# VectorE block transposes and a round trip through memory in place of TensorE transposes, in a fused windowed-attention and feed-forward kernel

## The reference

```python
# x: (4, 4096, 192), weight_gen: (4, 4096, 8 heads, 7 taps), moe_w_in: (192, 2048), moe_w_out: (2048, 192), all float32
w = softmax(weight_gen, axis=-1)                     # over the 7 taps, with 1e-9 added to the sum
attn[b, s, h, g] = sum_k w[b, s, h, k] * x_padded[b, s + k, h, g]   # x_padded: 6 zero rows ahead of each sequence
t = attn.reshape(16384, 192)
h = t @ w_in
out = (h * clip(h + 3, 0, 6) / 6) @ w_out
```

## Time and profile before

| what | value |
|---|---|
| three runs | 1182.89, 1185.61, 1186.64 us (median 1185.61) |
| the profiled execution | 1178.76 us, its span 1177.0 us |
| mean granted TensorE clock | 0.998 |
| busy: PE, PEld, DVE, ACT, POOL | 1162.3, 1089.3, 813.2, 662.0, 676.1 us |
| DMA | 42.34 MB, mean 36 GB/s |
| chain that ended last | PE 95% |

### The profile page before, as it was taken

One profiled execution on the slowest core, in us unless ns is written; L12 is line 12 of the kernel. 1 busy time (PEld: TensorE's weight loads), 2 busy tenths in 40 slices (PEclk: granted clock), 3 DMA queues, 4 the chain that ended last, 5 costly groups with the idle time before them and its releaser, 6 DMA issues.

```text
span 1177.0 us, 33989 instructions
## 1 busy us (share of the span) xinstructions
PE 1162.3 (99%) x13860; PEld 1089.3 (93%) x13860; DVE 813.2 (69%) x1359; ACT 662.0 (56%) x1273; POOL 676.1 (57%) x441
## 2 busy tenths in 40 slices
PE   8899999999999999999999999999999999999998
PEld 6899999999999999999999999999999999999997
DVE  7867767676766767767667676767667677676664
ACT  4555555565555555555555555556555565555554
POOL 5791854909459193682927639195590936829200
PEclk9999999999999999999999999999999999999999
DMA  6101010010100101010010100101001010100000
GB/s 188 48 23 62 23 62 0 21 60 21 60 0 25 56 21 60 20 47 14 21 60 21 47 13 21 60 21 60 0 21 60 21 60 16 47 18 13 14 14 15
DMA packets 12231, 42.34 MB, mean 36 GB/s; under 512 B 1199, under 2 KB 5295, under 8 KB 10283
## 3 DMA queue, kind: packets, MB, share of 16 engines
q1 hardware_dynamic: 12203, 41.93, 10.1%
HBM read 29.34 MB, written 12.58 MB: 36 GB/s over the span
## 4 chain that ended last, share of the span: by engine, by line
PE 95%; DVE 2%; DMA 1%; ACT 1%; SPq 1%; issue 0%; DVEq 0%; ACTq 0%
PE sums L599 34%; PE work L563 16%; PE sums L602 14%; PE work L577 13%; PE work L578 9%; PE work L564 8%; DMA w_in_raw<-moe_w_in_dram 1%; DVE g_lo L387 1%; PE work L528 0%; PE work L515 0%; DVE w_in L438 0%; ACT g_hi L288 0%; DVE work L382 0%; DVE w_out L444 0%; PE work L514 0%; DVE w_exp L362 0%
## 5 line engine op out<-in xcount | busy, mean ns | idle before, releaser
L599 PE MATMUL sums<-w_out,g_hi 64*128 64x384 f32 x4096 | 635.4, 355 | 3.5 <-DVE g_lo L387 2.9
L602 PE MATMUL sums<-w_out,g_lo 64*128 64x192 f32 x4096 | 545.1, 248 | 0.0
L382 DVE SCALAR_TENSOR_TENSOR work<-relu,work 128x512 f32<-128x512 f32 x512 | 331.2, 693 | 278.9 <-ACT relu L283 277.7
L283 ACT ACTIVATE relu<-work 128x512 f32<-128x512 f32 x512 | 279.4, 601 | 340.9 <-PE work L578 337.7
L599 PEld LDWEIGHTS sums<-w_out,g_hi 64*128 64x128 f32 x4096 | 424.8, 184 | 20.3 <-DVE g_lo L387 2.9
L602 PEld LDWEIGHTS sums<-w_out,g_lo 64*128 64x128 f32 x4096 | 430.0, 187 | 0.0
L288 ACT CAST g_hi<-work 128x512 fp32r<-128x512 f32 x512 | 300.7, 587 | 80.9 <-DVE work L382 78.2
L387 DVE TENSOR_TENSOR g_lo<-work,g_hi 128x512 fp32r<-128x512 f32 x512 | 330.3, 687 | 14.1
L189 POOL TENSOR_TENSOR pool_acc<-pool_acc,pool_prod 128x768 f32<-128x768 f32 x155 | 289.7, 1869 | 0.0
L182 POOL TENSOR_TENSOR pool_acc<-x_in,w_soft 128x768 f32<-128x768 f32 x31 | 48.8, 1573 | 417.1 <-DVE w_soft L376 405.3
L187 POOL TENSOR_TENSOR pool_prod<-x_in,w_soft 128x768 f32<-128x768 f32 x155 | 240.8, 1554 | 0.0
(11 more groups left out here) (60 smaller groups left out, 975.8 us busy)
## 6 DMA issues: line engine op xcount, KB each, us to landing
x_in<-x_dram SPq DMA_DIRECT2D x15, 1344.0 KB, 6.0
out_dram<-out_stage SPq DMA_DIRECT2D x32, 384.0 KB, 2.8
w_raw<-weight_gen_dram SPq DMA_DIRECT2D x16, 224.0 KB, 3.0
w_out_raw<-moe_w_out_dram SPq DMA_DIRECT2D x1, 1152.0 KB, 13.3
x_in<-x_dram SPq DMA_DIRECT2D x2, 384.0 KB, 5.3
w_in_raw<-moe_w_in_dram SPq DMA_DIRECT2D x1, 768.0 KB, 8.1
w_in_raw<-moe_w_in_dram SPq DMA_DIRECT2D x2, 384.0 KB, 10.0
w_out_raw<-moe_w_out_dram SPq DMA_DIRECT2D x1, 384.0 KB, 5.7
```

Source lines behind the costliest of these rows:

```text
L283: nc.scalar.activation(t.relu[:, m % 2, :], t.work[m % BANKS][:], ACT.Relu, bias=3.0).then_inc(s.relu_ready, 1)
L382: nc.vector.scalar_tensor_tensor(bank[:], t.relu[:, m % 2, :], 6.0, bank[:], ALU.min, ALU.mult).then_inc(s.gated, 1)
L599: nc.tensor.matmul(t.sums[n][:, 0:2 * D], t.g_hi[rows, m % G_SLOTS, n * P:(n + 1) * P], t.w_out[rows, j, :], start=(j == 0 and part == 0), ...
L602: ins = nc.tensor.matmul(t.sums[n][:, D:2 * D], t.g_lo[rows, m % G_SLOTS, n * P:(n + 1) * P], t.w_out[rows, j, 0:D], start=False, stop=las ...
```

## The change

The layout change leaves TensorE, except for the first half in the prologue. VectorE's `transpose` turns each 32x32 block of `attn_a` and `attn_b` into `blocks`; four transfers write `blocks` to a matrix `columns` (192 x 512) in memory (`spread`), and three read it back as `x_a` and (twice, for the two row groups of the array) `x_b` (`gather`). ScalarE rounds them (`x_hi`) and, but for the first two, GpSimd takes the remainder (`x_lo`), in its own queue. The transposing duo is gone: 8 duos to a half, 16 to a round. The columns of a half stand in another order, so a store is four transfers with pieces of 768 B (3,072 B in the first). A round is now 1,024 tokens of one sequence, partition p holding tokens 8p to 8p + 7, so that x and the halo come in three transfers. `G_SLOTS` goes from 6 to 8.

```diff
-GROUP_SLOTS = list(range(12)) + [TA, TB] + list(range(12, TILES))
-ROUND = 2 * SLOTS
+ROUND = 2 * TILES
-G_SLOTS = 6
+G_SLOTS = 8
-SHIFT_AT, EXP_AT, SUM_AT, SCALE_AT = 2, 3, 4, 5
+SHIFT_AT, EXP_AT, SUM_AT, SCALE_AT = (3, 2), (4, 3), (5, 4), (6, 5)
+SECOND_TURN_AT, SECOND_SPLIT_AT = 5, (7, 3)
+NEXT_TURN_AT, NEXT_SPLIT_AT = (12, 10), (15, 13)
+NEXT_SECOND_TURN_AT = (17, 16)
...
+    def load_x(q):
+        first = q * ROUND_TOKENS
+        sp.wait_ge(s.attn_ready, halves_attended(q - 1, 1))
+        sp.dma_start(t.x_in[1:P, :], tokens(dram.x, D, first + TOKENS - HALO, TOKENS + HALO, 1)).then_inc(s.x_loaded, 16)
+        sp.dma_start(t.x_in[0:1, HALO * D:], tokens(dram.x, D, first, TOKENS, 0, 1)).then_inc(s.x_loaded, 16)
+        before = tokens(dram.x, D, first - HALO, HALO, 0, 1) if q % PER_SEQUENCE else t.zeros[0:1, :]
+        sp.dma_start(t.x_in[0:1, 0:HALO * D], before).then_inc(s.x_loaded, 16)
+    def spread(q, half):
+        sp.wait_ge(s.turned_blocks, halves_attended(q, half))
+        sp.wait_ge(s.columns_loaded, LOADED * (2 * q + half - 1))
+        for b in range(BLOCKS):
+            sp.dma_start(bass.AP(dram.columns.tensor, b * P, [[N, BLOCK], [BLOCK * N, D // BLOCK], [1, P]]),
+                         t.blocks[BLOCK * b:BLOCK * (b + 1), :, :]).then_inc(s.columns_written, 16)
+    def gather(q, half):
+        sp.wait_ge(s.columns_written, WRITTEN * (2 * q + half))
+        sp.wait_ge(s.xt_lo_ready, inputs_split(q, half) - SPLIT_PARTS)
+        sp.dma_start(t.x_a[:], dram.columns[0:DA, :]).then_inc(s.columns_loaded, 16)
+        for lower in range(2):
+            sp.dma_start(t.x_b[lower * DB:(lower + 1) * DB, :], dram.columns[DA:D, :]).then_inc(s.columns_loaded, 16)
...
+    for q in range(PAIRS):
+        if q == 0:
+            spread(0, 1)
+            load_x(1)
+            gather(0, 1)
+        else:
+            spread(q, 1)
+            gather(q, 1)
+            store(q - 1, 1)
+        if q < PAIRS - 2:
+            sp.wait_ge(s.w_shifted, q + 2)
+            load_window_weights(q + 2)
         store(q, 0)
+        if q < PAIRS - 1:
+            spread(q + 1, 0)
+            gather(q + 1, 0)
+        if q < PAIRS - 2:
+            load_x(q + 2)
+    store(PAIRS - 1, 1)
...
+def x_hi(eng, t, s, q, half):
+    eng.wait_ge(s.columns_loaded, LOADED * (2 * q + half))
+    eng.copy(t.xt_a[:, half, 0, :], t.x_a[:]).then_inc(s.xt_hi_ready, 1)
+    eng.copy(t.xt_b[:, half, :], t.x_b[:]).then_inc(s.xt_hi_ready, 1)
+def x_lo(eng, t, s, q, half, by_one=False):
+    eng.wait_ge(s.xt_hi_ready, inputs_rounded(q, half))
+    eng.tensor_tensor(t.xt_a[:, half, 1, :], t.x_a[:], f32(t.xt_a[:, half, 0, :]), ALU.subtract).then_inc(s.xt_lo_ready, 1)
+    for odd in range(2):
+        if by_one:
+            eng.wait_ge(s.xt_lo_ready, inputs_split(q, half) - 2 + odd)
+        eng.tensor_tensor(block_b(t, half, odd, 1 - odd), blocks_of(t.x_b, odd, 1 - odd),
+                          f32(block_b(t, half, odd, 1 - odd)), ALU.subtract).then_inc(s.xt_lo_ready, 1)
...
     (GpSimd)
+    attend_next(0, 1, waits=False)
+    inputs_ready(1)
+    attend_next(1, 0, waits=False)
+    attend_next(1, 1)
+    with pool.Fori(1, PAIRS - 1) as q:
+        x_lo(nc.gpsimd, t, s, q, 1, by_one=True)
+        inputs_ready(q + 1)
+        attend_next(q + 1, 0)
+        attend_next(q + 1, 1)
+        x_lo(nc.gpsimd, t, s, q + 1, 0, by_one=True)
+    x_lo(nc.gpsimd, t, s, PAIRS - 1, 1, by_one=True)
...
     (ScalarE, in duo, behind relu and g_hi)
+        if d == SECOND_SPLIT_AT[not first]:
+            x_hi(nc.scalar, t, s, q, 1)
+        if d == EXP_AT[not first]:
             softmax_exp(q + 1)
+        if d == NEXT_SPLIT_AT[not first]:
+            x_hi(nc.scalar, t, s, q + 1, 0)
...
+    def turn(q, half):
+        dve.wait_ge(s.attn_ready, halves_attended(q, half))
+        dve.wait_ge(s.columns_written, WRITTEN * (2 * q + half - 1))
+        for attn, c0, c1 in ((t.attn_a, 0, DA), (t.attn_b, DA, D)):
+            nc.vector.transpose(t.blocks[:, c0 // BLOCK:c1 // BLOCK, :].rearrange("p e (n r) -> p n e r", r=BLOCK),
+                                attn[:, half, :].rearrange("p (n e c) -> p n e c", n=GT, c=BLOCK)
+                                ).then_inc(s.turned_blocks, 1)
     (VectorE, in duo, behind gate and g_lo)
+        if first and d == SECOND_TURN_AT:
+            turn(q, 1)
+        if first and d == SECOND_SPLIT_AT[0]:
+            x_lo(nc.vector, t, s, q, 1)
...
+        if d == NEXT_TURN_AT[not first]:
+            turn(q + 1, 0)
+        if first and d == NEXT_SPLIT_AT[0]:
+            x_lo(nc.vector, t, s, q + 1, 0)
+        if d == NEXT_SECOND_TURN_AT[not first]:
+            turn(q + 1, 1)
...
     (TensorE)
+    def fill_first(q, d):
+        if d % HALF_DUOS == 0:
+            pe.wait_ge(s.xt_lo_ready, inputs_split(q, d // HALF_DUOS))
```

More of the change, by code:

```diff
@@ L84, in turns_before, with inputs_split, inputs_rounded, halves_attended @@
     return 1 + 2 * (DUOS - 1) * q + 2 * (d - FIRST_DUO) + second_fill - ended
-def skipped(m, last):
-    return last and (m >= ROUND or (m >= SLOTS and not is_tile(m)))
 def tiles_done(q, m):
-    return 2 * TILES * q + sum(is_tile(i) for i in range(m + 1))
+    return ROUND * q + m + 1
 def duos_filled(q, d):
[L99 to L110, removed]
+    return DUOS * q + d + 1
+def inputs_split(q, half):
+    return SPLIT_PARTS * (2 * q + half + 1)
+def inputs_rounded(q, half):
+    return 3 + 2 * (2 * q + half)
+def halves_attended(q, half):
+    return 2 * (2 * q + half)
 def x_loads(q):
-    return 16 * X0_DMAS + 16 * q
+    return 16 * X_DMAS * (q + 1)
 def f32(ap):
@@ L238, in sync_program @@
-    for half in range(2):
[L239 to L242, removed]
-        store(q, 0)
[L244 to L248, removed]
-    for half in range(2):
-        sp.wait_ge(s.stored[half], 16 * PAIRS + 16)
+        first = (q * ROUND_TOKENS + half * GT) * D
+        for n in range(GT):
+            if q == 0 and half == 0:
+                to = bass.AP(dram.out.tensor, first + n * BLOCK * TOKENS * D, [[TOKENS * D, BLOCK], [1, GT * D]])
+            else:
+                to = bass.AP(dram.out.tensor, first + n * D,
+                             [[TOKENS * D, BLOCK], [BLOCK * TOKENS * D, BLOCKS], [1, D]])
+            sp.dma_start(to, t.out_stage[BLOCK * n:BLOCK * (n + 1), half, :]).then_inc(s.stored[half], 16)
@@ L288, in g_hi @@
         nc.scalar.copy(t.g_hi[:, m % G_SLOTS, :], t.work[m % BANKS][:]).then_inc(s.g_hi_ready, 1)
[L290 to L295, removed]
     def evacuate(q, half):
-        act.wait_ge(s.stored[half], 16 * q + 16)
+        act.wait_ge(s.stored[half], STORE * q + STORE)
         for n in range(GT):
@@ L304, in evacuate, with duo @@
                           1.0 / 6.0).then_inc(s.main_staged, 1)
-    def duo(q, d, last=False):
+    def duo(q, d, first=False, last=False):
         if d == HALF_DUOS + 1:
@@ L310, in duo @@
             evacuate(q, 1)
-        if skipped(2 * d, last):
+        if last and d >= DUOS:
             return
[L313 to L324, removed]
+        relu(q, 2 * d)
+        relu(q, 2 * d + 1)
+        g_hi(q, 2 * d)
+        g_hi(q, 2 * d + 1)
+        if d == SECOND_SPLIT_AT[not first]:
+            x_hi(nc.scalar, t, s, q, 1)
+        if last:
+            return
+        if d == EXP_AT[not first]:
             softmax_exp(q + 1)
+        if d == NEXT_SPLIT_AT[not first]:
+            x_hi(nc.scalar, t, s, q + 1, 0)
     def w_in_hi(group):
@@ L343, in scalar_program @@
     for d in range(FIRST_DUO + DUOS):
-        duo(0, d)
+        duo(0, d, first=True)
         if d < GROUPS - 1:
@@ L483, in tensor_program @@
 def tensor_program(nc, pe, t, s):
-    def transposes(half, what, bank, r):
-        src = t.attn_a if what == TA else t.attn_b
-        rows = ROWS[r]
-        return [(bank[:, i * P + r * DB:i * P + (r + 1) * DB], src[rows, half, i * P:(i + 1) * P], t.ident[rows, rows])
-                for i in range(GT if what == TA else GT // 2)]
     def transpose_tap(k):
@@ L745, with __init__ @@
 class Dram:
[L746 removed]
+    def __init__(self, x, weight_gen, moe_w_in, moe_w_out, out, columns):
         self.x = x
```

210 lines of the change are left out of this document (78 added, 132 removed).

## The result

The changed kernel takes 1833.82 us (median of 4 runs, 1832.85 to 1835.64), the kernel before in the same comparison 1184.25 us (median of 4, 1178.55 to 1186.64). The ratio is 1.550, with a 95% interval of 1.544 to 1.556. I had forecast 1271 us and a range up to 1305. The sign was right; some 563 us were missing.

The account below looks back on a forecast made before the run. TensorE's instruction stream, 99% busy, was taken as the bound. First round, GpSimd-bound rounds and end gave a 1251.3 us span, 1262.5 with clock; that is + 85.5 on the profiled execution, so 1185.6 + 85.5 = 1271 us, range 1243 to 1305.

Parts of the forecast that it names:

- the trip through memory: Columns written and read back in a steady round: 2.8 us landing each way, 1.6 us margin plus 2 us TensorE slack.
- Rival 2: Small-piece write and read of the columns are slow, ScalarE stands in `x_hi`: 2 us a round, 1299 us; chance 0.15.
- The loop of GpSimd: Steady rounds: fill, `w_soft`, two attentions, `x_lo`, next fill sum to 75.9 us; GpSimd needs 46.2 where 40.8 are available.
- The stall: TensorE waits for GpSimd's `x_lo` at a round's first fill, about 5.3 us in each of rounds 1 to 14.
- The signs: Expected profile: TensorE 92 to 93% busy, about 14 round waits and two first-round waits, GpSimd some 60% of the chain.
- Rival 3: GpSimd's stretch in the rounds is hidden behind TensorE, rounds 70.6 us apart: 1178 to 1185 us; chance 0.1.
- The clock: TensorE's clock drops at each stall: from nothing to 1.5 us, taken as 0.8 for each of 14 stalls.
- Rival 1: TensorE's clock pays in every stall: + 0.7 x 14 = 10 us, giving 1281 us; chance 0.2.
- The first round: Ahead of round 1, TensorE waits some 9 and 5 us; round 1's first fill starts at 104.1 us, before 91.7.
- The end: Last round's first gate to span's end: 77.2 us, plus 2.2 us for a last store of four issues and small pieces.
- The gain: Transposes leave TensorE: 0.55 us for each of 31 transposing duos, 17 us in all.

Follow-up runs that it names:

- e5: The changed kernel with the rounds' load of x queued behind the columns of half 1 instead of ahead of them; 1901.73 us, ratio 1.611.
- e1: The changed kernel with every load of x, prologue and rounds, cut into transfers of 112 and 15 partitions; 1296.31 us, ratio 1.098.
- e3: e1 with the softmax's sum and scaling moved up behind duo 3, so GpSimd's attentions start earlier; 1187.49 us, ratio 1.007.
- e9: e3 with its first round reworked: columns ahead of x, turns and splits earlier, half 1's first `x_lo` on GpSimd; 1177.90 us, ratio 0.9981.
- e4: The kernel before, with only each round's load of x split into 31 runs of 4 partitions and 1 run of 4; 1564.73 us, ratio 1.326.

## Why the prediction was wrong, step by step

**What failed.** One step, of which I wrote: "`load_x(q+2)` waits for the end of the attentions and is needed 30 us later, with 6.0 to land". The 6.0 us are of a transfer to 128 partitions. The change makes it one to 127, and the row of before has no such transfer. My own rule for operations that the trace doesn't show, bounds from both sides, was used on `x_lo`, on `turn` and on the trip through memory, and not on this load, since its bytes and its name had stayed. What the runs show in its place is a load on one DMA engine: about 52 us by its rate, 54.8 from issue to use in e5, 54.7 to the end of the write behind it here. The same figure was in the first round (columns "landing behind x's 1344 KB, 59.5"; ScalarE got them at 144.07, of which 35 us are the prologue's load, and at 62.70 in e1), and the prologue's load I did not cost at all.

**Rival 2 had the right place and the wrong cause.** ScalarE stood in `x_hi` of half 1 with the next relu behind it, as written there. I had 2 us for it; it was 33.9 us in the round shown and 53.8 at the most, and not from the small pieces: the page of the changed kernel has 2.0, 2.8 and 3.0 us as their median landings, and in e1 the wait is gone with the same pieces.

**The rest of the working, read in e1**, where the load is repaired and nothing else:
- *The loop of GpSimd.* From its start to TensorE's first fill, 299.90 to 346.00 in e1, 46.1 us; my sum was 46.2. `x_lo` took 1.26 + 1.52 = 2.8 us; I had 2.7 of 2.0 to 3.1. `turn` took 0.70 + 0.40 = 1.1 us, as taken. The stall is 5.0 us in e1; I had 5.3.
- *The signs.* TensorE was busy 92% in e1, with 14 waits in the rounds and two in the first, as written. GpSimd's share of the chain was 31% and not some 60%, and it stood idle 29 us in a round and not 20 to 25; between the attentions of two rounds it also waits for ScalarE's `x_hi` of half 1, which my sum left out and which cost nothing.
- *Rival 3's outcome.* e3 does not shorten GpSimd's stretch, which stays at 46.2 us; it starts the stretch earlier, and the rounds become 70.6 us, as that rival had them. It needed a change of the order that wasn't made.
- *The clock* was mis-sized. I took 0.8 us for each stall and 1.5 as the most. Here is e1 behind a stall:

```profile
346.00 0.79 PE L585 MATMUL work<-xt_a,w_in 64*128 64x512 f32 x1 [4.98 <-POOL xt_b L305]
```

```profile
346.00:347.00 1.00, 1.00 (x4) 0.83 (x6) 0.00 (x0) 0.00 (x0) 0.00 (x0) 0.50 1.00 312
347.00:349.00 2.00, 2.00 (x16) 1.78 (x14) 0.00 (x0) 0.00 (x0) 0.00 (x0) 0.50 0.88 215
349.00:351.00 2.00, 2.00 (x16) 1.88 (x14) 0.00 (x0) 0.00 (x0) 0.00 (x0) 0.50 0.13 27
351.00:352.00 1.00, 1.00 (x10) 0.78 (x8) 0.00 (x0) 0.00 (x0) 0.00 (x0) 0.68 0.00 0
352.00:353.00 1.00, 1.00 (x18) 1.00 (x16) 0.22 (x1) 0.85 (x2) 0.00 (x0) 1.00 0.00 0
```

  The granted clock is 0.50, the 1.2 GHz level, for more than 5 us after TensorE has begun again. The gate of the duo comes at 352.78, 6.8 us behind its fill in place of 4.24, and GpSimd's next start 32.3 us behind the fill in place of 29.7: 2.6 for each stall. Rival 1 was right in kind, and its price too small. I had argued that part of the low time falls into the stall; about 1 us did (0.91 from 344 to 345, 0.50 from 345 on), and more than 5 us of it came behind. Rounds of 78.4 us where the sum had 75.9 + 0.8 are 14 x 1.7 = 24 us of the 31 between the forecast's span and e1's, 1262.5 and 1293.8.
- *The first round* was 8.6 us later than I had it: the first duo of round 1 is gated at 116.91 in e1, where my sum has 108.3. VectorE's `x_lo` there, beside GpSimd, took 1.23 + 3.59 us for an estimate of 3.5, and the second stall was 4.3 where the sum had 4.6. The first was 15.1 for 9.
- *The end*: the clock and the first round are 32.4 us of a gap of 31.3, so the last round and the end together came out 1 us below the sum.

So of 563 us that were missing 538 are the one-engine load, and 25 (1296 less 1271) the clock and the first round. Those two are 31 us between the spans; the forecast's time stands 6 us closer by luck, since I had added 6.9 us for a median above the profiled execution, and e1's median is 0.7 above its own.

**The gain.** The 17 us from the transposing duos are real: e3's rounds against the kernel before's are 15 x 1.06 = 16 us shorter. They are less than what the first round and the end give back, until e9.

## What to carry to other kernels

When a change cuts a transfer, ask how its outermost dimension divides on either side, and cost it anew, even where the bytes stay: 127 partitions took about 52 us where 128 took 6.0, and with 112 + 15 the share is down to 0.13 from 349 on in e1, some 6 us behind the issue at 343.16. In a trace, read the busy share of the DMA engines inside the transfer before trusting what a row of the waits names; a share of 0.06 is one engine of 16, and the wait that it causes shows under other names (here the columns, ScalarE, VectorE). And where an engine's stretch is started by one instruction and awaited by another, the place of the starting instruction can be worth more than the stretch's length: 109 us here, for two entries moved by one duo and by two.

## What the hardware showed that I had not expected

- An issuing instruction can itself be held: the small transfer behind the big one kept SyncE 22.26 us in the changed kernel (in the next round it was the second small one, 23.21), and 22.29 us went to the two issues of x in a round of e4. What holds it there no run shows.
- With a stall of 5 us the granted clock was still 0.50 more than 5 us behind the restart (e1).
- Two subtractions of 64x256 on VectorE took 3.59 us beside GpSimd's attention and 0.87 us without it, in the same kernel (e1, first round):

```profile
65.13 3.59 DVE L305 TENSOR_TENSOR xt_b<-x_b,xt_b 64x256 fp32r<-64x256 f32 x2
...
108.89 0.87 DVE L305 TENSOR_TENSOR xt_b<-x_b,xt_b 64x256 fp32r<-64x256 f32 x2
```
